# The products of w_out's second layout with the routing matrices, spread over TensorE's early waits, in a language-model block on one Trainium2 core

## The reference

```python
# attention, per head and step t
m_new = max(f[t] + m, i[t]); f_stab = exp(f[t] + m - m_new); i_stab = exp(i[t] - m_new)
C = f_stab * C + i_stab * outer(v[t], k[t]);  n = f_stab * n + i_stab * k[t]
y[t] = sigmoid(o_gate[t]) * (C @ q[t]) / max(abs(n @ q[t]), 1)
# dense layers on x = y as [1536, 320]
g = softplus(x @ w_in);  x2 = g @ w_out
# experts
e = argmax(x2 @ w_gate);  p = softmax(x2 @ w_gate)[e];  s = sigmoid(x2 @ w_output_gate)[e]
out = p * s * (relu(x2 @ w1[e]) @ w2[e])
```

## Time and profile before

| what | us |
|---|---|
| median of 3 runs | 433.79 |
| fastest, slowest of them | 431.26, 436.87 |
| the profiled execution's own time | 433.11 |
| its span, first to last instruction | 431.4 |
| TensorE busy | 391.8 |
| VectorE, ScalarE, GpSimd busy | 283.2, 225.6, 210.3 |

### The profile page before, as it was taken

How to read it: one execution, slowest core, us unless ns; L and a number is a source line. 1 busy time by engine, 2 the same in 40 slices (tenths; PEclk the granted TensorE clock), 3 DMA queues, 4 the chain that set the end, 5 groups by cost and what they waited for, 6 DMA issues and landing times.

```text
span 431.4 us, 9562 instructions
## 1 busy us (share of the span) xinstructions
PE 391.8 (91%) x2763; PEld 363.2 (84%) x2764; DVE 283.2 (66%) x488; ACT 225.6 (52%) x405; POOL 210.3 (49%) x226
## 2 busy tenths in 40 slices
PE   0869997799999999999999999799999999989972
PEld 0728886689999999999999998788989988869872
DVE  8965999957757788555666676668564278573320
ACT  4714782464445555555556644716555269574320
POOL 5624897834645766333233372145364235746220
PEclk9866999899999999999999999899999999999998
DMA  7983576326255445645222210567573432921110
GB/s 195 338 367 122 167 220 196 133 77 180 71 160 181 163 115 164 192 113 184 70 68 68 69 49 1 178 255 271 193 272 82 168 126 85 359 83 53 36 43 16
DMA packets 30682, 63.43 MB, mean 147 GB/s; under 512 B 8984, under 2 KB 20763, under 8 KB 30012
## 3 DMA queue, kind: packets, MB, share of 16 engines
q1 hardware_dynamic: 28780, 57.61, 41.3%
q0 software_dynamic: 1808, 5.31, 3.7%
q10 hardware_dynamic: 64, 0.15, 0.1%
HBM read 56.40 MB, written 6.88 MB: 147 GB/s over the span
## 4 chain that ended last, share of the span: by engine, by line
PE 67%; DMA 8%; DVE 7%; issue 7%; POOL 4%; SPq 2%; ACT 2%; DVEq 1%; POOLq 0%; ACTq 0%
PE ps L1500 5%; PE ps L1502 5%; PE ps L1501 5%; PE ps L1484 4%; PE ps L1486 4%; PE ps L1485 4%; DMA wout_t<-w_out_t 4%; PE ps L1616 4%; PE ps L1618 4%; PE ps L1617 4%; PE ps L1590 3%; PE ps L1592 3%; PE ps L1591 3%; PE ps L1492 2%; PE ps L1491 2%
## 5 line engine op out<-in xcount | busy, mean ns | idle before, releaser
L1131 DVE SCALAR_TENSOR_TENSOR gsum<-ps,soft 128x384 f32<-128x384 f32 x64 | 35.6, 558 | 54.2 <-ACT soft L873 54.1
L865 ACT ACTIVATE soft<-ps 128x384 f32<-128x384 f32 x64 | 31.5, 492 | 69.1 <-PE ps L1492 69.0
L653 POOL TENSOR_TENSOR win_lo<-win_raw,win_hi 128x256 fp32r<-128x256 f32 x32 | 24.3, 760 | 84.7 <-DVE win_hi L1118 84.7
L1500 PE MATMUL ps<-wout_hi,ghi 128*128 128x336 f32 x192 | 61.0, 318 | 1.0 <-DVE glo L1137 1.0
L1502 PE MATMUL ps<-wout_hi,glo 128*128 128x336 f32 x192 | 60.6, 316 | 0.0
L1501 PE MATMUL ps<-wout_lo,ghi 128*128 128x336 f32 x192 | 60.6, 316 | 0.0
L1484 PE MATMUL ps<-xhi,win_hi 128*128 128x384 f32 x128 | 43.5, 340 | 1.4 <-DVE gsum L1131 0.8
L1486 PE MATMUL ps<-xhi,win_lo 128*128 128x384 f32 x128 | 43.2, 338 | 0.0
L1485 PE MATMUL ps<-xlo,win_hi 128*128 128x384 f32 x128 | 43.2, 337 | 0.0
L1616 PE MATMUL ps<-split,hthi 128*128 x120 | 38.3, 319 | 3.4 <-DVE htlo L1295 2.4
L1500 PEld LDWEIGHTS ps<-wout_hi,ghi 128*128 128x128 f32 x192 | 36.0, 188 | 1.7 <-issue 1.2
(11 more groups left out here) (207 smaller groups left out, 1005.9 us busy)
## 6 DMA issues: line engine op xcount, KB each, us to landing
e1raw<-w_e SPq DMA_DIRECT2D x24, 512.0 KB
e2raw<-w_e SPq DMA_DIRECT2D x16, 640.0 KB, 5.1
win_raw<-w_in SPq DMA_DIRECT2D x32, 192.0 KB, 2.5
wout_raw<-w_out SPq DMA_DIRECT2D x32, 160.0 KB, 2.1
kq<-kq_t SPq DMA_DIRECT2D x16, 240.0 KB
wout_t<-w_out_t SPq DMA_DIRECT2D x3, 1024.0 KB, 13.7
og<-o_t SPq DMA_DIRECT2D x2, 1152.0 KB, 17.5
kr<-k_rows SPq DMA_DIRECT2D x8, 240.0 KB, 4.7
```

The lines of the kernel that those rows point to most:

```text
L1131: dve.scalar_tensor_tensor(half(gsum, hf), ps[:, hf, 0:S // 2], 0.0, half(soft, hf), ALU.max, ALU.add).then_inc(g_done, 1)
L1500: pe.matmul(o, ghi[u][:, cols], wout_hi[u][:, :], start=False, stop=False, skip_group_check=True)
```

## The change

wout_t's parts get a semaphore each. The products of parts 0 and 1 move ahead of updates(0), those of part 2 stay behind the eleventh cast, and they all go to bank 6 instead of bank 3; the cast f(2,1) takes bank 3 for it, and f(2,2) stays in 7. The transposes move behind scores(1), in the loop's first turn, and the wait for w_route ahead of outputs(0). ScalarE copies route_t behind its reads of the first two d casts, and w_route behind carries(1). In SP's queue rows(2) and kq(3) come directly behind wout_t, with waits for its second and third part, then og 0, rows(3), kq(4), and only then w_in, w_out and og 1.

```diff
-    return f + [("d", 0, 0, 7), ("d", 0, 1, 4)] + [("f", 2, k, 5 + k) for k in range(3)]
+    return f + [("d", 0, 0, 7), ("d", 0, 1, 4)] + [("f", 2, k, (5, 3, 7)[k]) for k in range(3)]
...
+        wt_loaded = [sem(f"wt_loaded{k}") for k in range(KT)]
...
             for k in range(KT):
-                sp.dma_start(wout_t[:, k, :], w_out_t[:, k * F1:(k + 1) * F1]).then_inc(wt_loaded, 16)
+                sp.dma_start(wout_t[:, k, :], w_out_t[:, k * F1:(k + 1) * F1]).then_inc(wt_loaded[k], 16)
...
+            sp.wait_ge(wt_loaded[1], 16)
+            load_rows(2)
+            sp.wait_ge(wt_loaded[2], 16)
+            load_kq(3)
+            sp.dma_start(og[0][:, :, :], o_t[0]).then_inc(og_loaded[0], 16)
+            load_rows(3)
+            load_kq(4)
             for u in range(2):
                 load_in(u, u)
                 load_out(u, u)
-            for b in range(B):
-                sp.dma_start(og[b][:, :, :], o_t[b]).then_inc(og_loaded[b], 16)
-            load_rows(2)
-            load_kq(3)
-            load_rows(3)
-            load_kq(4)
+            sp.dma_start(og[1][:, :, :], o_t[1]).then_inc(og_loaded[1], 16)
             sp.wait_ge(w_route_done, 1)
...
-            act.wait_ge(wt_done, 1)
-            nc.scalar.copy(route_t[:, :], ps[:, 3, :]).then_inc(route_t_done, 1)
-            act.wait_ge(route_turned, 1)
-            nc.scalar.copy(w_route[:, :, :]..., ps[:, 3, :]...).then_inc(w_route_done, 1)
+            def early_weights():
+                act.wait_ge(wt_done, 1)
+                nc.scalar.copy(route_t[:, :], ps[:, 6, :]).then_inc(route_t_done, 1)
+            def turned_weights():
+                act.wait_ge(route_turned, 1)
+                nc.scalar.copy(w_route[:, :, :]..., ps[:, 6, :]...).then_inc(w_route_done, 1)
             def iteration(j):
                 for cast in casts_of(j)[:2]:
                     read_cast(*cast)
+                if j == 0:
+                    early_weights()
...
                 if j + 1 < PAIRS:
                     carries(j + 1)
+                if j == 0:
+                    turned_weights()
...
+            def route_weights(k):
+                pe.wait_ge(wt_loaded[k], 16)
+                for j in range(4):
+                    last = pe.matmul(ps[32 * j:32 * j + 32, 6, :], wroute[:, k, :], wout_t[:, k, j * F1 // 4:(j + 1) * F1 // 4],
+                                     start=(k == 0), stop=(k == KT - 1))
+                if k == KT - 1:
+                    last.then_inc(wt_done, 1)
...
             for it in first[8:10]:
                 cast(*it)
+            pe.wait_ge(route_w_loaded, 32)
+            pe.wait_ge(cast_read, CASTS["f", 1, 2])
+            route_weights(0)
+            route_weights(1)
             pe.wait_ge(cast_read, CASTS["f", 2, 0])
             updates(0)
             cast(*first[10])
...
-            route_weights()
-            turn_route_weights()
+            route_weights(KT - 1)
             pe.wait_ge(d_split, 1)
-            pe.wait_ge(w_route_done, 1)
             for j in range(PAIRS):
                 casts = casts_of(j)
                 if j + 1 < PAIRS:
                     for it in casts[:2]:
                         cast(*it)
                     scores(j + 1)
+                    if j == 0:
+                        turn_route_weights()
                     for it in casts[2:4]:
                         cast(*it)
                     updates(j + 1)
                 if j == 0:
                     pe.wait_ge(cast_read, len(first))
+                    pe.wait_ge(w_route_done, 1)
                 outputs(j, casts[4] if len(casts) > 2 else None)
```

More of the change, by code:

```diff
@@ L303, in build_program @@
         mm2_done, x2_act, x2_dve = sem("mm2_done"), sem("x2_act"), sem("x2_dve")
-        wt_loaded, wt_done, route_t_done, route_turned, w_route_done = sem("wt_loaded"), sem("wt_done"), sem("route_t_done"), sem("route_turned"), sem("w_route_done")
+        wt_loaded = [sem(f"wt_loaded{k}") for k in range(KT)]
+        wt_done, route_t_done, route_turned, w_route_done = sem("wt_done"), sem("route_t_done"), sem("route_turned"), sem("w_route_done")
         logits_copied = sem("logits_copied")
@@ L826, in _ @@
                     carries(0)
-            act.wait_ge(wt_done, 1)
-            nc.scalar.copy(route_t[:, :], ps[:, 3, :]).then_inc(route_t_done, 1)
-            act.wait_ge(route_turned, 1)
-            nc.scalar.copy(w_route[:, :, :].rearrange("p (j m) r -> p m j r", j=4), ps[:, 3, :].rearrange("p (m j r) -> p m j r", m=4, j=4)[:, :, :, 0:2 * E]).then_inc(w_route_done, 1)
+            def early_weights():
[3 more added lines that the diff above has]
+                act.wait_ge(route_turned, 1)
+                nc.scalar.copy(w_route[:, :, :].rearrange("p (j m) r -> p m j r", j=4), ps[:, 6, :].rearrange("p (m j r) -> p m j r", m=4, j=4)[:, :, :, 0:2 * E]).then_inc(w_route_done, 1)
             def iteration(j):
@@ L1418, in outputs, with turn_route_weights @@
                 last.then_inc(pv_done, 1)
+            def route_weights(k):
[5 more added lines that the diff above has]
+                    last.then_inc(wt_done, 1)
+            def turn_route_weights():
+                pe.wait_ge(route_t_done, 1)
+                for m in range(4):
+                    last = pe.transpose(ps[:, 6, m * P:(m + 1) * P], route_t[:, m * P:(m + 1) * P], identity)
+                last.then_inc(route_turned, 1)
             pe.wait_ge(pick_done, 1)
```

## The result

The changed kernel takes 428.77 us (median of 4 runs, 427.7 to 429.8) against 433.27 us before (4 runs on the same chip, 431.26 to 436.87): a ratio of 0.987, 95% interval 0.983 to 0.991. That is 4.5 us less, and within 2%. The forecast was 427.8. The profiled execution took 428.29 us, 4.8 less than the 433.11 of before; its span is 426.5 against 431.4.

What follows compares the result with a forecast made beforehand. TensorE was taken to bound the kernel, with a gap before the loop over pairs and 3.03 us of slow clock in pair 0. The earlier start and a clock rise near 29 gave 6.0: 433.79 - 6.0 = 427.8 us, range 423.8 to 432.0.

Steps and rivals of the forecast that it cites:

- The gap at the start: TensorE before the loop over pairs: products start as each third lands, so the loop begins 4.2 us sooner, at 27.2.
- I take 0: Transfers at the start: wout_t lands no sooner with the new queue; 2.4 us kept for the range.
- Transposes and copies: Transposes moved behind scores(1) cost their 0.66 us and no wait; ScalarE's copies, moved too, cause no wait.
- VectorE: Later updates(0) cost states(0) at most 0.1 us; scans(2) are a floor, so weigh(1) can't start before 29.0.
- The clock in pair 0: Start of the loop: clock rises at about 29, pair 1 starts at about 35.0 against 41.0, 6.0 us gained.
- rival 2: Clock back before the loop, or wout_t sooner: gain 7.3 to 8.5, up to 10; 425.3 to 426.5 us; chance 0.25.
- nothing said of the clock: Start of the kernel: net gain of the moved products, transposes and copies without any clock effect, 3.6 us.
- I pass the gain on in full: Everything behind pair 1 runs as before, only sooner, so the whole 6.0 us reaches the end.
- Queue: SP's new order of loads costs nothing; og 0 over 3 us late would hold back pair 2's d casts.
- 1 (clock low through pair 0): Clock rises only by pair 1, so the gain is 2.6 us; time 431.2 us; chance 0.22.
- 3 (low beyond): Clock stays at 0.50 beyond pair 0, 3.0 us per further slow pair; 437.3 us; chance 0.04.
- 4 (given back later): Sooner start lost later to VectorE's slack or ScalarE's gate waiting for og; 433.8 us; chance 0.05.

Runs made afterwards that it cites:

- engines_only: Changed kernel with SP's old queue, keeping the new order of TensorE, ScalarE and banks; 428.79 us, ratio 0.989 to the kernel before.
- after: First profile of the changed kernel, nothing further edited; profiled execution 428.29 us, span 426.5.
- turn_early: Changed kernel with the transposes and ScalarE's two copies put back ahead of the loop over pairs; 429.48 us, ratio 0.990 to the kernel before.
- kq2_late: Changed kernel with wout_t issued ahead of kq(2), pair 2's k and q loads; 428.81 us, ratio 0.986 to the kernel before.
- after_nudged: Changed kernel with four small memsets on GpSimd ahead of v for pair 6; 428.9 us, ratio 0.989 to the kernel before.
- before_again: The kernel before, unchanged, profiled once more; 434.19 us in its one execution, span 432.5.
- after_again: The changed kernel, unchanged, run and profiled once more; 428.7 us, ratio 0.987 to the kernel before, span 424.9.
- The nudges: Four small memsets added on VectorE to the kernel before (433.06 us, ratio 0.999), and on GpSimd to the changed kernel (428.9 us, ratio 0.989).
- one_group: Changed kernel with all three thirds' products together again behind updates(0) and the eleventh cast; 432.7 us, ratio 0.996 to the kernel before.
- late_filled: Changed kernel with fifteen products of zeros on TensorE ahead of the last pair's scores; 429.22 us, ratio 0.990 to the kernel before.
- queue_only: Kernel before with only SP's queue in the new order; 433.76 us, ratio 1.000 to the kernel before.

## Why the prediction was right, and where its terms were off

- **The gap at the start: right.** Forecast: products at 19.3 and 21.7, the third without a wait, loop at 27.2. Measured: 20.42, 22.79, no wait, 26.86. The thirds landed 1 us later than in the profile of before, and the clock, which had risen for updates(0) and the last third, gave that back. That the queue isn't the cause of the later landing is seen in runs with the old queue and with the new one: the first products wait until 19.64 in engines_only, 20.42 in after and 18.71 in turn_early. The medians from issue to landing are 13.7 to 14.4 us in five profiles with the old queue and 13.0 to 14.9 in eight with the new one (kq2_late left out): the "I take 0" of the prediction holds.
- **Transposes and copies: right.** 0.66 us, no wait; turn_early puts the removed waits at 0.71 and 0.51 (0.70 and 0.55 were taken).
- **VectorE: right.** weigh(1) at 29.33 (29 to 30). Updates(0) later cost it 0.58 of waiting, not 0.1, inside slack. Its floor, which the prediction named, is what kq2_late ran into.
- **The clock in pair 0: the term that was mis-sized.** Rise forecast at 29, measured at 24.5; 6.0 us forecast at pair 1, 7.2 measured. By that step alone rival 2 came true (7.3 for a rise at 25.8). The Trainium skill's rule on the page "TensorE: Matmul & The Clock Gate", Part 1 (activity releases the throttle), which gave the 7.3 there, was nearer than my reading of 32.5 to 36.0. But neither is a constant of the kernel: in after_nudged, the same instructions up to there, the clock rose at about 28.3 and pair 1 began at 35.23, as the forecast laid out (29 and 35.0). And the prize itself was half an accident: the 3.03 us of slow clock in pair 0 were one execution's, and before_again doesn't have them. With the clock alike on both sides the forecast's own 3.6 ("nothing said of the clock") stands against 3.75 and 4.7 measured (2.3 with after_nudged).
- **"I pass the gain on in full": not quite.** 7.2 at pair 1, 6.2 at the sums, 6.4 at the last slot, 4.9 of span. What took 1.0 of it up to the sums: pair 1 to pair 5 are 0.2 longer in after, and from pair 5 to the sums it takes 24.2 us against 23.4, with the 3.38 us wait for p_w and a low clock behind it. The port lock doesn't explain that: v won it in after and lost it in before. What took 1.5 more is the clock in the last slot (5.32 against 3.78, in after but not in after_again). Against before_again the same kernel's gain grows, from 3.75 at pair 1 to 6.0 of span. The forecast's 6.0 was an oversized term passed on undiminished; the medians say 4.5 here and 5.4 on another chip. That 427.8 lies 1 us from the 428.77 measured is in part luck: the forecast gain at pair 1 was 1.2 too low for this profile, and 2.3 were lost behind it where no loss was forecast, and both hang on the execution.
- **Queue: right in sum.** Worth nothing that the median shows; the 1.25 us that it saves at pair 2's rows I hadn't seen, nor the 0.59 for og.
- **Rivals.** 1 (clock low through pair 0) and 3 (low beyond) didn't come. 4 (given back later) holds for a third of the 7.2 us, by other waits than the two that it named. One sum of rival 3 was off: with three further slow pairs it gives 433.8 - 2.6 + 9.1 = 440.3, which is 1.5% slower; over 2% takes four.
- **Open:** how often each way of the port lock, of pair 0's clock and of the last slot's clock comes up in unprofiled executions, and so what each is worth to the median; nor does any run show why the clock at the start rises at 24.5 us in after and at 28.3 in after_nudged. The nudges turned the lock in their profiles and left the times where they were; whether they turned it in all executions is not seen. Why one_group's median (432.7) lies only 1.6 us under before, with a pair 1 0.6 us sooner than before_again's, fits the scatter but isn't shown.

## What to carry to other kernels

A block of work that waits for a transfer in pieces is worth splitting by piece and putting into the engine's existing idle time; here that, not the queue, was 3 to 4 us of the 4.5 to 5.5. Before a slow clock or a wait in one stage is booked as a prize, a second profile of the same kernel should show it too: here a 3.0 us prize and a 1.5 us loss came and went between executions of identical code, and pair 5 took 5.43 us in after and 10.42 in late_filled, whose edit comes only behind it. And a start can only be pulled forward until the next engine's own schedule is the floor: 4.7 us more won at the loop's start (kq2_late) were gone one pair later.

## What was not expected of the hardware

- Two small loads ahead of a large one can cost more than their bytes. kq(2) is 0.5 MB on 40 partitions, some 1.2 us at the 418 GB/s of the earlier trace rows. With it ahead of wout_t the median third takes 14.9 us from issue to landing in after and 13.0 to 14.8 in the twelve other profiles, without it 10.7: 2.3 to 4.2 us. That rests on the one profile of kq2_late. While wout_t is the last load under way in after (up to 22.76), some of the DMA engines are idle:

```profile
19.00:21.70 2.70, 1.28 (x8) 0.23 (x8) 2.67 (x2) 0.73 (x2) 1.71 (x1) 0.50 0.70 291
```

  The page "DMA: Bandwidth & Descriptors" of the Trainium skill, section "Why a DMA increments its semaphore by 16 and not by 1", has the rule that puts a transfer of 40 partitions on 10 of 16 engines, with which the share of 0.70 agrees roughly.
- The landing of the same transfers moves between executions: first third at 18.7 to 20.4 us with the same queue.
- TensorE's clock can be low where the profile's clock column shows 1.00. In queue_only and one_group the d_row casts take 2.92 us instead of 1.56, and in queue_only the 24 products take 5.34 us, at a clock column of 1.00, as this window of queue_only shows. The durations decide. In queue_only the column stays at 1.00 up to 33 us, in one_group up to 66, so a mean clock taken over such a span is too high.

```profile
25.30:31.00 5.70, 5.34 (x24) 1.10 (x24) 4.03 (x3) 0.29 (x1) 0.76 (x2) 1.00 0.81 249
```

- The race for the port between GpSimd and VectorE is decided by a few tenths of a microsecond (leads of 0.10 to 0.21 us lost, 0.28 and more won). Pair 5 takes 5.4 us with v won and 7.9 to 10.4 with v lost. In the two nudged kernels 1.4 to 2.2 us of that are left a stage later, and none in the medians.
